# A delta-rule attention kernel: the scaling of the inverse blocks split between DVE and ACT, with corner and loads reordered

## The reference

```python
B, H, S, D = q.shape                       # 4, 8, 768, 48
k_n = k / (np.linalg.norm(k, axis=-1, keepdims=True) + 1e-06)
state = np.zeros((B, H, D, D))
for t in range(S):
    kt, vt, bt = (k_n[:, :, t], v[:, :, t], beta[:, :, t, None])
    y[:, :, t] = np.einsum('bhd,bhde->bhe', q[:, :, t], state)
    v_old = np.einsum('bhde,bhd->bhe', state, kt)
    state = state + bt[..., None] * np.einsum('bhd,bhe->bhde', kt, vt - v_old)
```

## Time and profile before

| what | value |
|---|---|
| runs of the kernel (3) | 862.98, 866.08, 870.26 us, median 866.08 |
| profiled execution | 862.98 us, span 861.1 us, mean granted clock of PE 0.986 |
| first `corner` | 32.96 us from the span's start |
| last output copied, dense part begins | about 272 us |
| busy in the span | PE 788.0, PEld 550.6, DVE 516.6, ACT 319.8, POOL 161.6 us |

### The profile page before, as it was taken

How to read it: one execution, slowest core, us unless ns; L and a number is a source line. 1 busy time by engine, 2 the same in 40 slices (tenths; PEclk the granted TensorE clock), 3 DMA queues, 4 the chain that set the end, 5 groups by cost and what they waited for, 6 DMA issues and landing times.

```text
span 861.1 us, 24818 instructions
## 1 busy us (share of the span) xinstructions
PE 788.0 (92%) x10976; PEld 550.6 (64%) x10976; DVE 516.6 (60%) x1212; ACT 319.8 (37%) x635; POOL 161.6 (19%) x195
## 2 busy tenths in 40 slices
PE   5588788888786999999999999999999999999998
PEld 4588788888785456665666556665656666665654
DVE  5997879786842774633364236455555767758522
ACT  3355466555442252222222223322342444433211
POOL 5232223221100100300030001002121423323200
PEclk9699999999998999999999999999999999999999
DMA  8134333322102132010001000000000000000001
GB/s 202 50 84 129 95 77 78 78 59 59 41 23 60 62 112 81 1 56 1 28 28 43 13 29 28 1 1 2 1 1 1 1 29 20 19 19 28 30 27 56
DMA packets 45048, 37.70 MB, mean 44 GB/s; under 512 B 27401, under 2 KB 39052, under 8 KB 44940
## 3 DMA queue, kind: packets, MB, share of 16 engines
q1 hardware_dynamic: 38020, 30.95, 12.8%
q10 hardware_dynamic: 6920, 5.15, 2.2%
HBM read 26.65 MB, written 4.72 MB: 36 GB/s over the span
## 4 chain that ended last, share of the span: by engine, by line
PE 81%; DVE 8%; issue 5%; ACT 3%; DMA 1%; SPq 1%; POOL 0%; DVEq 0%; ACTq 0%
PE bank L292 15%; PE bank L1014 6%; PE bank L1062 5%; PE bank L1060 5%; PE bank L1016 5%; PE bank L1061 5%; PE bank L1015 5%; PE bank L998 3%; PE bank L1000 3%; PE bank L999 3%; PE bank L324 2%; PE bank L948 2%; PE bank L954 2%; DVE hT_lo L1432 2%; PE bank L347 1%
## 5 line engine op out<-in xcount | busy, mean ns | idle before, releaser
L1180 ACT ACTIVATE hT_hi<-bank 128x384 f16<-128x384 f32 x96 | 46.7, 488 | 160.9 <-PE bank L1000 160.7
L1432 DVE SCALAR_TENSOR_TENSOR hT_lo<-bank,hT_hi 128x384 f16<-128x384 f32 x96 | 53.3, 556 | 73.6 <-ACT hT_hi L1180 73.3
L1014 PE MATMUL bank<-wA,hT_hi 128*128 128x384 f16 x288 | 94.1, 327 | 2.8 <-DVE hT_lo L1432 2.8
L998 PE MATMUL bank<-unT,wA 128*128 128x384 f16 x288 | 94.1, 327 | 0.3 <-DVE hT_lo L1432 0.3
L1000 PE MATMUL bank<-unT,wA 128*128 128x384 f16 x288 | 94.0, 326 | 0.0
L999 PE MATMUL bank<-unT,wA 128*128 128x384 f16 x288 | 94.0, 326 | 0.0
L1016 PE MATMUL bank<-wA,hT_lo 128*128 128x384 f16 x288 | 94.0, 326 | 0.0
L1015 PE MATMUL bank<-wA,hT_hi 128*128 128x384 f16 x288 | 94.0, 326 | 0.0
L292 PE MATMUL bank<-Yv,ET 64*64 64x48 f32 x2304 | 76.4, 219 | 9.7 <-issue 7.2
L292 PEld LDWEIGHTS bank<-Yv,ET 64*64 64x64 f32 x2304 | 73.3, 135 | 13.0 <-issue 8.7
L430 ACT ACTIVATE Yv<-bank,rows 128x384 f32<-128x384 f32 x72 | 40.5, 577 | 67.5 <-PE bank L292 67.3
(11 more groups left out here) (198 smaller groups left out, 1679.0 us busy)
## 6 DMA issues: line engine op xcount, KB each, us to landing
Kb<-k_dram SPq DMA_DIRECT2D x24, 192.0 KB, 4.0
Vv<-v_dram SPq DMA_DIRECT2D x12, 384.0 KB, 4.5
z_first<-w_dram SPq DMA_DIRECT2D x8, 576.0 KB, 4.0
z_first<-wt_dram SPq DMA_DIRECT2D x8, 576.0 KB, 3.7
out_dram<-hT_hi SPq DMA_DIRECT2D x24, 192.0 KB, 1.9
KQ<-q_dram SPq DMA_DIRECT2D x44, 96.0 KB, 3.4
X<-Yo ACTq DMA_DIRECT2D x12, 192.0 KB
X<-Yo ACTq DMA_DIRECT2D x10, 189.0 KB
```

What stands on the lines that cost most here:

```text
L998: pe.matmul(out, w1[0][:, k, cols], unT[0][:, k, :], start=(k == 0), stop=False)
L1014: pe.matmul(out, hT[0][:, f, cols], w2[0][:, f, :], start=(f == 0), stop=False)
L1180: act.activation(hT[0][:, f, :], bank[3 + m % 3][:, 0:TG * P], ACT.Relu).then_inc(s_hh, 1)
L1432: dve.scalar_tensor_tensor(hT[1][:, f, :], bank[3 + m % 3][:, 0:TG * P], 0.0, hT[0][:, f, :], ALU.max, ALU.subtract).then_inc(s_hl, 1)
```

## The change

Six edits, all in `attention`:

1. The spread of U over two columns of blocks moves from DVE to ACT: `scaled_u` becomes one multiply into a new tile `Us`, and a new ACT function `spread` copies Us twice into Ux, masked. In `blocks_in` the sum of two halves becomes two masked instructions.
2. `Dy`, `To` and `cd` are laid out with the pair index outside the group index. The transposes then read and write in order; `placed` reads To in the order g, x, i from a tile laid out i, x, g. `rows` has 7 columns for 11.
3. On PE `corner(c, 0)` comes ahead of `predicted(c)`, and `direct(c, 0)` ahead of `grow(c)`.
4. On ACT `root` comes ahead of `grown`; the order then is grown(c), spread(c+1), output 0, placed(c+1), output 1.
5. On DVE `mask_e(c, 0)` comes ahead of `make_x(c)`; `blocks_in` is for c + 1 and ahead of its elimination; norm or scale stand between `scaled_u` and `blocks_out`; for c = -2 scale(0) stays where it was.
6. On SP the load of Q waits for the products of hop 1, and the load of K for those of hop 3.

```diff
-        Dy = sb("Dy", [P, BLK, NG, 2])
+        Dy = sb("Dy", [P, BLK, 2, NG])
-        To = sb("To", [P, NG, 2, BLK])
+        To = sb("To", [P, BLK, 2, NG])
+        Us = sb("Us", [P, BLK, BLK])
...
                 load_v(c + 2 if c + 2 > 1 else -1)
+                if c >= 0:
+                    sp.wait_ge(s_Y, 8 * c + 4)
                 load_q(c + 3 if c + 3 > 2 else -1)
+                if c >= 0:
+                    sp.wait_ge(s_Y, 8 * c + 8)
                 load_k(c + 5 if c + 5 > 3 else -1)
...
             for c in range(C0, NC):
+                corner(c, 0)
                 predicted(c)
-                corner(c, 0)
                 corner(c, 1)
...
                 out = queried(c)
+                direct(c, 0, out)
                 grow(c)
-                direct(c, 0, out)
                 direct(c, 1, out)
...
                 for x in range(2):
-                    copy(Dy[:, :, :, x], Ab[:, n % RA, :, BLK * x:BLK * (x + 1)].rearrange("p g j -> p j g"),
-                         scale=rows[:, 5 + x:6 + x]).then_inc(s_hb, 1)
+                    copy(Dy[:, :, x, :], Ab[:, n % RA, :, BLK * x:BLK * (x + 1)].rearrange("p g j -> p j g"),
+                         scale=rows[:, 5:6]).then_inc(s_hb, 1)
+
+            def spread(n):
+                if not there(n):
+                    return
+                act.wait_ge(s_us, n + 1)
+                if n:
+                    act.wait_ge(s_to, n)
+                for x in range(2):
+                    copy(Ux[:, :, x, :], Us[:], scale=rows[:, 3 + x:4 + x]).then_inc(s_sp, 1)
...
-                    copy(TT[:, :, 2 * BLK * y:2 * BLK * (y + 1)], To[:].rearrange("p g x i -> p g (x i)"),
-                         scale=rows[:, 9 + y:10 + y]).then_inc(s_tt, 1)
+                    copy(TT[:, :, 2 * BLK * y:2 * BLK * (y + 1)].rearrange("p g (x i) -> p g x i", x=2),
+                         To[:].rearrange("p i x g -> p g x i"), scale=rows[:, 5 + y:6 + y]).then_inc(s_tt, 1)
...
                 copied_y(c, 3)
-                grown(c)
-                placed(c + 1)
-                output(c, 0)
-                output(c, 1)
                 if c % 2:
                     root((c + 3) // 2)
+                grown(c)
+                spread(c + 1)
+                output(c, 0)
+                placed(c + 1)
+                output(c, 1)
                 store(c)
...
-                dve.tensor_tensor(Rb[:], Tt[:, :, 0, :], Tt[:, :, 1, :], ALU.add).then_inc(s_in, 1)
+                dve.tensor_scalar(Rb[:], Tt[:, :, 0, :], rows[:, 3:4], None, ALU.mult).then_inc(s_in, 1)
                 dve.wait_ge(s_in, at + 4)
+                dve.scalar_tensor_tensor(Rb[:], Tt[:, :, 1, :], rows[:, 4:5], Rb[:], ALU.mult, ALU.add).then_inc(s_in, 1)
...
-                for x in range(2):
-                    dve.scalar_tensor_tensor(Ux[:, :, x, :].rearrange("p i k -> p k i"), U[:], rows[:, 3 + x:4 + x], by, ALU.mult,
-                                             ALU.mult).then_inc(s_us, 1)
+                dve.tensor_tensor(Us[:].rearrange("p i k -> p k i"), U[:], by, ALU.mult).then_inc(s_us, 1)
...
-                dve.transpose(To[:].rearrange("p g x i -> p i (g x)"), Ux[:].rearrange("p i x k -> p i (x k)")).then_inc(s_to, 1)
+                dve.transpose(To[:].rearrange("p i x g -> p (i x g)"), Ux[:].rearrange("p i x k -> p i (x k)")).then_inc(s_to, 1)
...
             for c in range(C0, NC):
+                mask_e(c, 0)
                 make_x(c)
-                mask_e(c, 0)
                 mask_e(c, 1)
-                eliminate(c + 1, (1, 2, 3, 4, 5, 6, 7, 8, 9, 10, 11, 12, 13, 14))
+                blocks_in(c + 1)
+                eliminate(c + 1, (1, 2, 3, 4, 5, 6, 7))
+                if c < 0 and c % 2 == 0:
+                    scale((c + 2) // 2)
+                eliminate(c + 1, (8, 9, 10, 11, 12, 13, 14))
                 scaled_u(c + 1)
-                blocks_out(c + 1)
                 if c % 2:
                     norm((c + 3) // 2)
-                else:
+                elif c >= 0:
                     scale((c + 2) // 2)
-                blocks_in(c + 2)
+                blocks_out(c + 1)
```

More of the change, by code:

```diff
@@ L68, in constants @@
     mU = np.broadcast_to(upper.reshape(1, BLK * BLK), (P, BLK * BLK))
-    x, y, odd = (p // BLK) % 2, (p // (2 * BLK)) % 2, p % 2
-    rows = np.concatenate([t[:, None] // BLK == np.arange(3)[None, :], odd[:, None] == np.arange(2)[None, :],
-                           (2 * y + x)[:, None] == np.arange(4)[None, :], y[:, None] == np.arange(2)[None, :]], 1)
+    z = (p // BLK) % 4
+    rows = np.concatenate([t[:, None] // BLK == np.arange(3)[None, :], z[:, None] % 2 == np.arange(2)[None, :],
+                           z[:, None] // 2 == np.arange(2)[None, :]], 1)
     return {
@@ L115, in attention @@
         mU = sb("mU", [P, BLK * BLK])
-        rows = sb("rows", [P, 11])
+        rows = sb("rows", [P, 7])
         bt = sb("bt", [P, NC * NG])
@@ L119, in attention @@
         ms = sb("ms", [P, 2, 2 * NG])
-        cd = sb("cd", [P, 2, NG, 2])
+        cd = sb("cd", [P, 2, 2, NG])
         cx = sb("cx", [P, 2, 2, BLK])
@@ L134, in attention @@
         s_in, s_iv = sem("block_steps"), sem("inverse_steps")
-        s_hb, s_us, s_to, s_tt = sem("upper_blocks"), sem("inverse_scaled"), sem("inverse_turned"), sem("TT_made")
+        s_hb, s_us, s_sp, s_to, s_tt = (sem("upper_blocks"), sem("inverse_scaled"), sem("inverse_spread"), sem("inverse_turned"),
+                                        sem("TT_made"))
         s_e, s_et = sem("E_product"), sem("E_masked")
@@ L202, in attention @@
         STEPS = 2 + 28
-        IN = 5
+        IN = 6
         NS = 11
@@ L558, in scale @@
                 if pair >= 2:
-                    dve.wait_ge(s_us, 2 * (2 * pair - 2))
+                    dve.wait_ge(s_us, 2 * pair - 2)
                 m = ms[:, pair % 2, :]
-                both = [P, 2, NG, 2]
+                both = [P, 2, 2, NG]
                 steps = [
@@ L570, in scale @@
                     lambda: dve.tensor_tensor(
-                        cd[:], nr[:, 5, :].rearrange("p (n g) -> p n g", n=2).unsqueeze(3).broadcast_to(both),
-                        bt[:, 2 * pair * NG:2 * (pair + 1) * NG].rearrange("p (n g) -> p n g", n=2).unsqueeze(3).broadcast_to(both),
+                        cd[:], nr[:, 5, :].rearrange("p (n g) -> p n g", n=2).unsqueeze(2).broadcast_to(both),
+                        bt[:, 2 * pair * NG:2 * (pair + 1) * NG].rearrange("p (n g) -> p n g", n=2).unsqueeze(2).broadcast_to(both),
                         ALU.mult),
-                    lambda: dve.transpose(cx[:].rearrange("p n x i -> p (n x i)"), cd[:].rearrange("p n g x -> p (n g x)")),
+                    lambda: dve.transpose(cx[:].rearrange("p n x i -> p (n x i)"), cd[:].rearrange("p n x g -> p (n x g)")),
                     lambda: dve.tensor_scalar(cT[:, pair % 2], cx[:, :, 0, :], rows[:, 3:4], None, ALU.mult),
@@ L589, in blocks_in @@
                     dve.wait_ge(s_hb, 2 * n + x + 1)
-                    dve.scalar_tensor_tensor(Dy[:, :, :, x],
+                    dve.scalar_tensor_tensor(Dy[:, :, x, :],
                                              Ab[:, n % RA, :, BLK * (x + 2):BLK * (x + 3)].rearrange("p g j -> p j g"),
-                                             rows[:, 7 + x:8 + x], Dy[:, :, :, x], ALU.mult, ALU.add).then_inc(s_in, 1)
+                                             rows[:, 6:7], Dy[:, :, x, :], ALU.mult, ALU.add).then_inc(s_in, 1)
                 dve.wait_ge(s_in, at + 2)
-                dve.transpose(Tt[:].rearrange("p j x i -> p (j x i)"), Dy[:].rearrange("p j g x -> p (j g x)")).then_inc(s_in, 1)
+                dve.transpose(Tt[:].rearrange("p j x i -> p (j x i)"), Dy[:].rearrange("p j x g -> p (j x g)")).then_inc(s_in, 1)
                 dve.wait_ge(s_in, at + 3)
@@ L626, in scaled_u @@
                 if n:
-                    dve.wait_ge(s_to, n)
+                    dve.wait_ge(s_sp, 2 * n)
                 by = cT[:, (n // 2) % 2, n % 2, :].unsqueeze(2).broadcast_to([P, BLK, BLK])
-                for x in range(2):
-                    dve.scalar_tensor_tensor(Ux[:, :, x, :].rearrange("p i k -> p k i"), U[:], rows[:, 3 + x:4 + x], by, ALU.mult,
-                                             ALU.mult).then_inc(s_us, 1)
+                dve.tensor_tensor(Us[:].rearrange("p i k -> p k i"), U[:], by, ALU.mult).then_inc(s_us, 1)
             def blocks_out(n):
@@ L635, in blocks_out @@
                     return
-                dve.wait_ge(s_us, 2 * n + 2)
+                dve.wait_ge(s_sp, 2 * n + 2)
                 if n:
                     dve.wait_ge(s_tt, 2 * n)
-                dve.transpose(To[:].rearrange("p g x i -> p i (g x)"), Ux[:].rearrange("p i x k -> p i (x k)")).then_inc(s_to, 1)
+                dve.transpose(To[:].rearrange("p i x g -> p (i x g)"), Ux[:].rearrange("p i x k -> p (i x k)")).then_inc(s_to, 1)
             def mask_e(n, u):
```

5 lines of the change are left out of this document (3 added, 2 removed).

## The result

The changed kernel takes 908.61 us (median of 4 runs, 906.07 to 910.19) against 868.17 for the kernel before: a ratio of 1.047, 95% interval 1.041 to 1.053. It is 40 us slower. The forecast had said 33 us slower, 896 us, with a range up to 908. The direction and the place were right, the size too small.

What follows compares the result with a forecast made beforehand. PE was taken as the bound, with the placing chain newly exposed between chunks. 11 transitions x (3.8 - 1.1) = 29.7, plus 2.9 at the start, gave +33 us on 862.98: 896 us, range 876 to 908.

Steps and rivals of the forecast that it cites:

- The chain named in the prediction: Between hop 3 and the next chunk's solve: grow, grown, spread, transpose, placed, corner in series; 10.6 us against 6.86, +3.8 per chunk.
- corner's wait: Before each chunk's first corner, PE would stand idle for about 4 us, waiting for ACT's TT.
- The 0.51: ACT's spread, between grown and DVE's transpose: 0.51 us taken for each copy of 256 elements, 0.93 for the overlapping pair.
- the loads behind SP's waits: On SP, the V load, tables at c = 2 and last store stand behind the new waits; nothing would be late.
- Scale, free of POOL's squares: On DVE, scale took 5.9 us beside POOL's squares; with K later POOL is idle there, so it was costed at nothing.
- rival 4: In the attention loop, PE's 4 us idle per chunk might lower the clock: +2 a chunk, +22, 918 us; chance 0.07.
- the gaps given back: PE's instruction-packet gaps in the attention loop fall from 2.7 to 1.3 us plus 0.3 for load collisions: -1.1 per chunk.
- the start: Between chunk 0's elimination and the first corner, the new chain takes 6.6 us against 3.7: +2.9 us.

## Why the prediction was right in its place and wrong in its size

**Right.** The chain named in the prediction is the one in the trace: grow, grown, spread, transpose, placed, corner. Its links came out close: spread 0.504 each (0.51 taken), To 0.710 (0.711), Us 0.594 (0.6), TT 1.154 (1.19), corner's wait 3.6 to 4.8 us in ten of eleven chunks (about 4). The 0.51 used a rate of 0.82 ns per element that the prediction does not name; ACT's 504 and 713 ns for 256 and 512 elements in the runs give just that. With a step of 128 bytes in what it reads ACT's copy took 1.154 us, and 0.713 with the step taken out of the read. The access-pattern rule of the Trainium skill ("SBUF — State Buffer", the section on the DMA port swizzle) is that each access that crosses into a new 16-byte line pays a penalty, and here the trace agrees. None of the loads behind SP's waits held up an engine that a run shows; what the tables' burst behind them did is told above. Scale, free of POOL's squares, took 2.94 us in place of 5.9 and lay in cover:

```profile
147.88 0.16 DVE L579 TENSOR_SCALAR nr<-nr 128x32 f32<-128x32 f32 x1
...
150.57 0.25 DVE L592 SCALAR_TENSOR_TENSOR cT<-cx,rows,cT 128x32 f32<-128x32 f32 x1
```

**Wrong: the clock was left out of the sum.** The step that failed is the weighing of rival 4. It was priced about rightly, at 22 us, but given a chance of 0.07 and left out of the forecast, because the kernel before held 1.00 with PE idle 15% of the stretch "in pieces of 1 us". The argument held for that trace's pieces of 1 us and said nothing about one piece of 4; the rows about long pieces, 272 to 280 us with 0.72 and the first corner at 3.68 us behind 9.44 of idle, spoke for the rival. What the runs showed in its place: the granted clock in the loop fell to 0.90, and behind the waits the 64x64 matmuls ran at half pace. The Trainium skill ("TensorE: Matmul & The Clock Gate", "HAM oscillation") describes a loop in which TensorE waits for data once per tile and so starts every tile at the lower clock; the trace agrees with it behind most of the eleven waits, and the prediction did not weigh that page. By PE's busy time the clock takes about 17 us in the loop of the profiled execution, and 14 to 16 us come back when the idle is filled. The dense part, from the last output's copy to the end of the span, took some 3 us more, 590.9 us against 588.0. Its first 20 us ran at a lower clock in the changed kernel (second line) than in the one before (first line), 0.66 against 0.83; why is not shown.

```profile
273.00:293.00 20.00, 13.46 (x38) 6.40 (x39) 11.51 (x21) 3.49 (x6) 0.00 (x0) 0.83 0.25 79
```

```profile
314.00:334.00 20.00, 13.68 (x27) 5.64 (x28) 9.70 (x19) 3.31 (x5) 0.00 (x0) 0.66 0.26 79
```

**Too small: the gaps given back.** The forecast took 1.1 us per chunk, within bounds of 0 to 2.7. The waits before corner stand in one group of the page of the changed kernel:

```profile
L298 PE MATMUL bank<-TT,AP 64*64 64x64 f32 x768 | 40.4, 281 | 55.3 <-issue 55.3
```

Less the 12.2 of the start, the eleven in the loop sum to 43.1 us. The remaining idle in the stretch is 56.4 - 43.1 - 0.8 (the end of the starting wait) = 12.5 us, against 35.7: 23.2 less, or 2.1 per chunk. With the waits cut to 13.5 us by PE's old order the rest rose to 23.6; filling the wait with 24 transposes brought other gaps back in part (1.02 us inside one grow, 0.47 inside one solve), and the loads' pacing moved nothing. So the gaps shrink where PE waits or is slowed anyway; how much of that is the idle and how much the slower matmuls behind it no run separates. That packets of instructions which come late are the cause of the gaps is argued from their places, in the middle of runs of matmuls, and from the 3.39 and 2.59 us gaps that stood just behind the tables' loads wherever these were put; no run changed the packets themselves. The Trainium skill ("Runtime: NRT & Kernel Launch", "Instruction fetch mechanics") says that the cost of refills is mostly hidden; the changed kernel, with 12.5 us of such gaps, comes nearer to that than the kernel before, which disagrees with 35.7 us of idle.

**Too small: the start**, 3.9 us for 2.9.

With the measured sizes the sum closes: 43.1 - 23.2 + 3.9 = 23.8 us, 17.3 for the clock, and 2.9 in the dense part make 44, the difference of the profiled executions (906.9 and 862.98). The forecast had 41.8 - 12.1 + 2.9 = 32.6 with nothing for the last two. Two errors of opposite sign, 11 us too little given back by the gaps and 17 us (20 with the dense part) left out for the clock, put the forecast some 12 us low. That it came so close is luck: with the gaps sized right and the clock still left out it would have said 885.

The share of the parts, by undoing each alone in the changed kernel: PE's order 24.6, spread's place 18.9, the clock 16 (by filling the wait), To's layout 6.7, SP's waits -3, the last two not clear of noise. They sum to more than the 40 us lost, since most of them shorten the same wait, and a shorter wait tends to cost less clock.

## What to carry to other kernels

When a step is moved to another engine, find what it now stands behind in that engine's queue, and then what the engine that sets the end still has to do meanwhile; here 0.9 us of harmless ACT work, queued behind the copy that waits for grow, put itself, the transpose and the placing in the open, and PE's new order took away the work that would have hidden part of them: a wait of 4 us. Price an idle stretch of TensorE twice: once as idle, and once for the matmuls behind it at the lower clock, by the rows that show what the clock did after the longest idle already in the trace. And put an access pattern's wide step on the side that is off the path: the change took 0.37 us off a DVE transpose and put 0.88 us on two ACT copies that were waited for.

## What the runs showed of the hardware

- With single idle pieces of about 4 us in each chunk the mean granted clock of the loop fell to 0.90, with PE busy 80% of the stretch (221.6 of 278 us). With the waits filled down to 0.3 to 1.2 us it was 0.99. With waits of 0.8 to 2.2 us it was 0.94, and with 2.2 to 4.6 us 0.90. A single wait's length did not tell what followed: 64 matmuls took 3.50 us behind 0.98 us of idle and 2.08 behind 1.23, and 30 of them took 1.09 us, full pace, behind a wait of 3.25 in the kernel with spread ahead of grown.
- PE's idle time outside the waits for TT shrank as these waits grew: 23.6 us with 13.5 us of waits, 12.5 us with 43.1, and with the data loads' pacing taken out it stayed there (56.5 us of idle in all, against 56.4).
- PE stopped for 2.6 to 3.4 us in the middle of a run of matmuls, with no semaphore there, just behind a burst of table loads; in the longest case the DMA engines were busy throughout (1.00, 324 GB/s).
- blocks_in, moved beside POOL's mask_p, met POOL there in most chunks: its two multiplies with two operands in SBUF took 754 and 739 ns on the mean, against 425 and 433 ns in the loop of the kernel before. In the changed kernel they took 0.92 to 0.94 and 0.84 us where mask_p ran beside them, and 0.42 and 0.43 where it did not. It was in cover and cost nothing that is seen.
